# Two searches of a mixture-of-experts kernel placed anew around its first expert

## The reference, cut to what matters

```python
logits = x @ w_gate                      # 3072 tokens, 8 experts
order = np.argsort(-flat)                # all (token, expert) scores, best first
for idx in order:                        # greedy, 384 tokens for each expert
    ...
for e in range(E):
    h = np.maximum(x[mask] @ w1[e], 0.0)     # 320 -> 1024
    out[mask] = h @ w2[e]                    # 1024 -> 320
h = x @ w_in                             # 320 -> 2048
g = np.where(h > 0.0, h, np.exp(np.minimum(h, 0.0)) - 1.0)
return g @ w_out                         # 2048 -> 320
```

## Time and profile before

| | us |
|---|---|
| median of three executions | 812.0 |
| the three | 810.54, 812.0, 812.1 |
| the profiled execution | 811.09 |
| its span in the trace | 809.3 |
| PE, DVE, ACT, POOL busy | 784.3, 520.8, 469.7, 397.2 |
| first expert, layer 1 from block 2 on | 210.07 to 239.96 |
| first expert, layer 2, with blocks 0 and 1 of the second | 239.96 to 295.27 |

### The profile page before, as it was taken

The page is one execution under the profiler, slowest core; times in us unless marked ns, Lnnn a source line. Parts: engine busy times, 40 slices in busy tenths (PEclk is TensorE's granted clock), DMA queues, the critical chain, the costliest instruction groups (busy, mean ns, idle before and its releaser), DMA issues.

```text
span 809.3 us, 17760 instructions
## 1 busy us (share of the span) xinstructions
PE 784.3 (97%) x6063; PEld 727.4 (90%) x6063; DVE 520.8 (64%) x1433; ACT 469.7 (58%) x1003; POOL 397.2 (49%) x472
## 2 busy tenths in 40 slices
PE   8999999999999999999999999999999999999995
PEld 7989898877789989999899999999998999999894
DVE  8667676867669747765865776576658656442441
ACT  7455555412428844882776288448727762993663
POOL 7545555534605750763365166517634651674243
PEclk9999999999999999999999999999999999999998
DMA  8999999333411311222021212112220212221000
GB/s 130 164 152 163 169 169 171 76 95 115 120 47 31 91 41 46 71 60 76 26 65 48 71 48 72 49 41 72 65 70 26 71 48 65 57 63 40 2 1 24
DMA packets 137763, 60.96 MB, mean 75 GB/s; under 512 B 104472, under 2 KB 135960, under 8 KB 137688
## 3 DMA queue, kind: packets, MB, share of 16 engines
q1 hardware_dynamic: 135208, 52.10, 29.7%
q0 software_dynamic: 2464, 7.89, 3.1%
q10 hardware_dynamic: 16, 0.01, 0.0%
HBM read 51.67 MB, written 8.26 MB: 74 GB/s over the span
## 4 chain that ended last, share of the span: by engine, by line
PE 64%; ACT 5%; DVE 4%; POOL 2%; issue 2%; DMA 1%; SPq 1%; ACTq 0%; POOLq 0%
PE bank L1950 7%; PE bank L2045 7%; PE bank L1951 6%; PE bank L1957 6%; PE bank L2047 6%; PE bank L2046 6%; PE bank L1959 3%; PE bank L1958 3%; PE bank L2003 3%; PE bank L2005 3%; PE bank L2004 3%; PE bank L1883 2%; PE bank L1991 1%; PE bank L1988 1%; ACT unit L1803 1%
## 5 line engine op out<-in xcount | busy, mean ns | idle before, releaser
L1359 POOL TENSOR_TENSOR gl_lo<-unit,gl_hi 128x384 fp32r<-128x384 f32 x128 | 130.5, 1020 | 266.3 <-ACT gl_hi L1819 266.1
L2045 PE MATMUL bank<-Wo_hi,gl_hi 128*128 128x320 f32 x384 | 124.8, 325 | 0.6 <-POOL gl_lo L1359 0.6
L2047 PE MATMUL bank<-Wo_hi,gl_lo 128*128 128x320 f32 x384 | 118.6, 309 | 0.0
L2046 PE MATMUL bank<-Wo_lo,gl_hi 128*128 128x320 f32 x384 | 118.3, 308 | 0.0
L1783 ACT ACTIVATE hid_hi<-bank 128x384 fp32r<-128x384 f32 x64 | 31.4, 490 | 129.0 <-PE bank L1959 129.0
L1622 DVE SCALAR_TENSOR_TENSOR unit<-bank,unit 128x384 f32<-128x384 f32 x104 | 57.9, 556 | 73.7 <-ACT bank L1812 73.7
L1800 ACT ACTIVATE unit<-bank 128x384 f32<-128x384 f32 x128 | 62.2, 486 | 49.6 <-PE bank L1959 40.5
L1950 PE MATMUL bank<-x_hi,Wi_hi 128*128 128x384 f32 x224 | 80.2, 358 | 2.4 <-DVE unit L1625 1.6
L1951 PE MATMUL bank<-x_hi,Wi_lo 128*128 128x384 f32 x224 | 75.8, 338 | 0.0
L2045 PEld LDWEIGHTS bank<-Wo_hi,gl_hi 128*128 128x128 f32 x384 | 72.5, 189 | 3.1 <-POOL gl_lo L1359 3.1
L1625 DVE TENSOR_TENSOR unit<-unit,bank 128x384 f32<-128x384 f32 x128 | 70.9, 554 | 4.4
(11 more groups left out here) (301 smaller groups left out, 2098.7 us busy)
## 6 DMA issues: line engine op xcount, KB each, us to landing
stage<-in_moe_w_dram SPq DMA_DIRECT2D x32, 320.0 KB, 2.9
stage<-in_moe_w_dram SPq DMA_DIRECT2D x32, 256.0 KB, 2.6
stage<-in_moe_w_dram SPq DMA_DIRECT2D x96, 64.0 KB, 2.4
k_in<-in_k_dram SPq DMA_DIRECT2D x24, 160.0 KB, 3.8
q_in<-in_q_dram SPq DMA_DIRECT2D x24, 160.0 KB, 4.4
o_in<-in_o_gate_dram SPq DMA_DIRECT2D x24, 160.0 KB, 4.0
v_in<-in_v_dram SPq DMA_DIRECT2D x24, 160.0 KB, 3.6
x_rows<-xt SPq DMA_DIRECT2D x24, 160.0 KB, 3.2
```

Of the source, the lines that this page charges most:

```text
L1359: nc.gpsimd.tensor_tensor(gl_lo[:, b, :], ex[:, b, :], gl_hi[:, b, :].bitcast(F32), ALU.subtract).then_inc(gl_ok, 1)
L2045: nc.tensor.matmul(acc[j][:, 0:DM], gl_hi[:, f % RG, t_], Wo_hi[:, f, :], start=(f == 0), stop=False)
L2046: nc.tensor.matmul(acc[j][:, 0:DM], gl_hi[:, f % RG, t_], Wo_lo[:, f, :], start=False, stop=False)
L2047: return nc.tensor.matmul(acc[j][:, 0:DM], gl_lo[:, f % RG, t_], Wo_hi[:, f, :], start=False, stop=(f == NF2 - 1))
```

## The change

It concerns the first expert alone; it gets a `first_body` of its own on VectorE and on PE, and what the general `body` had for it is deleted.

- Layer 1: each round q = 2 to 6 of the second search lies over block u = q. The threshold product of round u - 1 stands between `up_high(u)` and `up_low(u)`, the count of round u between the first and the second column block of `down(u - 2)` (for which `down` is split into `down_begin` and `down_block`), the fold behind `down`. There are no filler products. `totals` and both `prefix` move to block 7, behind `down(0, 6)` and behind `down(0, 7)`. On VectorE `choose_expert` and `choose_ties` come behind `hidden(0, 7)`, and `choose_leave` and `choose_close` behind `between_layers`.
- Layer 2: `choose_spots` at blocks 0 to 3, `choose_start(2)` at block 4, `list_tokens(1)`, `choose_tokens(1)` and `choose_keys(2)` at block 5, the slices two by two at blocks 6, 7 and 8. The third search goes by half blocks (2f ahead of `down2`, 2f + 1 behind it): round 1 counts at half 21 with its threshold at half 22, and from half 24 on each round has three halves. Round 6 stands at halves 36 and 37, around `down2(0, 15)`. VectorE makes the search's steps ahead of `elu` of the block, and those of round 6's test after `hidden(1, 1)`.

```diff
-    SLICES_BESIDE_SPOTS = {0: (0,), 2: (1,), 4: (2,), 5: (3, 4), 6: (5,)}
+    SLICES_BEHIND_LIST = {6: (0, 1), 7: (2, 3), 8: (4, 5)}
+    LIST_BESIDE, FIRST_LIST_BESIDE = 0, 5
+    def step_beside(half):
+        if half < 24:
+            return {21: (1, 1), 22: (1, 2)}.get(half, (0, 0))
+        return 2 + (half - 24) // 3, (half - 24) % 3
...
@@ VectorE @@
+        def third_search(half):
+            q, part = step_beside(half)
+            if q == 1:
+                if part == 1:
+                    round_test(2, 1)
+                else:
+                    round_move(2, 1)
+                    round_compare(2, 2)
+            elif q in FOLDED:
+                if part == 0:
+                    round_parts(2, q)
+                elif part == 1:
+                    round_test(2, q)
+                else:
+                    round_move(2, q)
+                    round_compare(2, q + 1)
+            elif q == ROUNDS and part == 0:
+                round_test(2, q)
+        def first_body():
+            round_test(1, 1)
+            round_move(1, 1)
+            round_compare(1, 2)
+            hidden(0, 2)
+            for q in range(2, ROUNDS):
+                round_parts(1, q)
+                round_test(1, q)
+                round_move(1, q)
+                round_compare(1, q + 1)
+                hidden(0, q + 1)
+            round_test(1, ROUNDS)
+            round_move(1, ROUNDS)
+            choose_counts(1)
+            hidden(0, NF - 1)
+            choose_expert(1)
+            choose_ties(1)
+            between_layers(0)
+            choose_leave(1)
+            choose_close(1)
+            for f in range(NF2):
+                third_search(2 * f)
+                third_search(2 * f + 1)
+                elu(0, f)
+                if f < SPOTS:
+                    choose_spots(1, f)
+                elif f == SPOTS:
+                    choose_start(2)
+                if f == FIRST_LIST_BESIDE:
+                    choose_tokens(1, 1, 0)
+                    choose_keys(2)
+                for part in SLICES_BEHIND_LIST.get(f, ()):
+                    compare_first(2, part)
+                if TURN <= f < TURN + NJ:
+                    columns(1, f - TURN)
+            for step in range(2):
+                third_search(2 * (NF2 + step))
+                third_search(2 * (NF2 + step) + 1)
+                hidden(1, step)
+            third_search(2 * (NF2 + 2))
+            round_move(2, ROUNDS)
...
@@ TensorE @@
+            elif q in FOLDED:
+                (count_parts, fold_parts, count_thresholds)[part](2, q)
+        def first_body():
+            for u in range(2, NF):
+                up_high(0, u)
+                if u == 2:
+                    count_takers(1, 1)
+                else:
+                    count_thresholds(1, u - 1)
+                up_low(0, u)
+                if u == 2:
+                    count_thresholds(1, 1)
+                down_begin(0, u - 2)
+                if u in FOLDED:
+                    count_parts(1, u)
+                elif u == ROUNDS:
+                    count_takers(1, u)
+                else:
+                    totals(1)
+                down_block(u - 2, 1)
+                if u in FOLDED:
+                    fold_parts(1, u)
+            down(0, NF - 2)
+            prefix(1, 1, eqs)
+            down(0, NF - 1)
+            prefix(1, 2, mem)
+            for f in range(NF2 + LAG):
...
+                third_search(2 * f)
+                if f >= LAG:
+                    down2(0, f - LAG)
+                third_search(2 * f + 1)
+                if f == FIRST_LIST_BESIDE:
+                    list_tokens(1)
+                if TURN <= f < TURN + NJ:
+                    columns(1, f - TURN)
+                if NF2 <= f < NF2 + 2:
+                    up(1, f - NF2)
```

More of the change, by code:

```diff
@@ L1659, in body @@
         def body(k, s, n, after):
+            if first_expert(k):
+                return first_body()
             c = k + 1
             for u in range(2, NF):
[L1663 to L1698, removed]
@@ L1712, in body @@
                 hidden(k, u)
-            if after == 2 and not first_expert(k):
+            if after == 2:
                 choose_start(c + 1)
@@ L1736, in body @@
                     round_test(c + 1, q)
[L1737 removed]
+                if after and f == LIST_BESIDE:
                     choose_tokens(c, 1 - s, n + s)
                 if after == 2:
[L1740 removed]
+                    for part in SLICES_BESIDE.get(f, ()):
                         compare_first(c + 1, part)
[L1742 to L1747, removed]
+                    if f == COUNT_BESIDE:
+                        round_test(c + 1, 1)
                 if TURN <= f < TURN + NJ and after:
                     columns(c, f - TURN)
[L1750 to L1756, removed]
+            if after:
                 hidden(c, 0)
@@ L1978, in up, with down_begin @@
             up_low(k, f)
[L1980 removed]
+        def down_begin(k, f):
             if f == 0:
@@ L2000, in down, with down_block @@
                 ins.then_inc(mid_pe, 1)
[L2001 to L2008, removed]
+            down_block(f, 0)
+        def down_block(f, c):
+            first, last, b, a = f == 0, f == NF - 1, f % HR, c * P
+            nc.tensor.matmul(acc[c][:, 0:CAP], W2[:, f, a:a + P], hid_hi[:, b, :], start=first, stop=False)
+            nc.tensor.matmul(acc[c][:, 0:CAP], W2[:, f, DM + W3 + a:DM + W3 + a + P], hid_hi[:, b, :], start=False, stop=False)
+            ins = nc.tensor.matmul(acc[c][:, 0:CAP], W2[:, f, a:a + P], hid_lo[:, b, :], start=False, stop=last)
+            if last:
+                ins.then_inc(mid_pe, 1)
+            elif c == 1:
                 ins.then_inc(down_pe, 1)
+        def down(k, f):
+            down_begin(k, f)
+            down_block(f, 1)
         def up2(k, f):
@@ L2139, in body @@
                 elif 1 < f < NF2:
-                    if f == LAG and after and not first_expert(k):
+                    if f == LAG and after:
                         list_tokens(c)
```

62 lines of the change are left out of this document (23 added, 39 removed).

## The result

The changed kernel takes 814.3 us in the median of 20 runs (811.6 to 818.7), the kernel before 811.9 us (809.7 to 815.6, 20 runs): a ratio of 1.0030, 95% interval 1.0018 to 1.0043. It is slower by 0.3%; forecast were 809.6 us, 0.3% faster. The profiled execution of after had 814.04 us with a span of 812.3 us, 3.0 us longer than that of before.

What follows compares the result with a forecast made beforehand. PE was taken as the bound, with only avoidable work and waits to win. Layer 1 -3.25, between the layers +0.15 and layer 2 +1.25 sum to -1.85, say -1.9 us: from 811.5 to 809.6 us, range 807.0 to 811.6.

Steps and rivals of the forecast that it cites:

- The waits that appear: Layer 1, blocks 2 to 4: PE waits for VectorE's compares and casts, 0.4, 0.2, 0.3 and 0.1, sum 1.0 us.
- 8.35 - 3.1: Layer 1: 8.35 us of search rounds and slower first products go out, 3.1 us of split small products come back.
- The hold of L1435: Layer 1, block 4: VectorE step held by POOL's split of weight piece 6, delaying compare and count, +1.0 us.
- rival 1: One of two large holds (L1435 in block 4, elu of block 14) is missed: 808.5 us, chance 0.25.
- Between the layers: From layer 1 to layer 2: moved choose steps on VectorE cost PE 0 to 0.6 us, taken as 0.15.
- The weight pieces: Layer 1: the nearest piece is ready 1.0 us before PE wants it, so no wait.
- step (a): Layer 2, blocks 4 and 5: moved key steps held beside POOL for 3 us, 0.4 us of it reaching PE.
- (b): Layer 2, block 16: PE waits 0.5 us at round 4's threshold and 0.8 us for round 5's compare.
- (c): Layer 2, block 14: elu held 1.1 us by POOL's split of piece 5; PE's fold of round 4 waits 1.3.
- The forecast for layer 2: Waits of 1.75 us go, 3.0 us come from key-step holds, block 16 and block 14: net +1.25 us.
- Rival 4: VectorE becomes the bound of blocks 12 to 15, five all-SBUF steps each held 1.1 us: 814.0 us, chance 0.05.
- The sign given for "wrong": Sum wrong if layer 1 gives under 2.5 us, holds are absent, or PE waits over 4 us in blocks 12-16.

Runs made afterwards that it cites:

- layer1_alone: Layer 1 as in the changed kernel, layer 2 and third search as in the kernel before; 811.56 us against 811.06 for before, ratio 1.0004.
- gather_block6: The changed kernel with POOL's three gathers one block earlier (blocks 6 to 8); 809.77 us against 811.53 for the kernel before, ratio 0.9980.
- keys_unheld: The changed kernel with the key steps of blocks 4 and 5 given a PSUM operand; 809.75 us against 811.06 for before, ratio 0.9989.
- after_again: The changed kernel itself, timed again beside the kernel before; 813.65 us against 811.06, ratio 1.0029.
- layer2_alone: Layer 1 as in the kernel before, layer 2 and third search as in the changed kernel; 817.40 us against 811.06 for before, ratio 1.0075.
- fillers_in_wait: The changed kernel with 16 filler products on PE ahead of the count of half block 27; 812.90 us against 811.53 for before, ratio 1.0011.
- split4_later: The changed kernel with POOL's split of weight piece 4 one block later; 812.77 us against 811.53 for the kernel before, ratio 1.0014.
- unheld_split5: keys_unheld with POOL's split of weight piece 5 one block later; 809.08 us against 811.53 for the kernel before, ratio 0.9968.
- gather6_split5: gather_block6 with POOL's split of weight piece 5 one block later; 807.44 us against 811.60 for the kernel before, ratio 0.9955.

## Why the prediction was wrong

**Layer 1: right, but for one hold.** A block with a folded round takes 3.40 us in after (from 222.39 to 225.79), a block without any small product took 2.80 in before (from 233.95 to 236.75): 0.60 for a round, near the 0.57 read from the earlier trace rows. The waits that appear came to about 1.1 us (0.4 and 0.1 in block 2, 0.4 in block 3, 0.2 in block 4) for 1.0 forecast. 8.35 - 3.1 - 1.1 = 4.15, measured 4.14; so close a fit is luck, since the same layer 1 took from 24.50 to 25.45 us in the ten traces that have it (L1; 24.87 in after). The hold of L1435, taken as met at +1.0, was missed:

```profile
220.30 0.18 DVE L1435 SCALAR_TENSOR_TENSOR lo<-hi,lo 128x24 f32<-128x24 f32 x1
...
220.58 1.29 POOL L1067 TENSOR_TENSOR W_split<-stage,W_split 128x512 fp32r<-128x512 f32 x1 [1.20 <-ACT W_split L1051]
```

It is done 0.1 us before POOL starts. In layer1_alone, the same code, the transfers came elsewhere, L1433 took 0.97 and L1435 0.39, and the count waited 0.95. The margin was named (0.2 us), and that is all that can be said of such a hold beforehand; rival 1 (one of the two large holds missed) is what came in layer 1. Between the layers nothing was lost, for 0.15 forecast: from the last product of layer 1 to the first of layer 2 it is 0.47 us in both. The weight pieces cost nothing, as forecast.

**Layer 2, step (a): the size right, the consequence wrong.** The holds of the key steps came to 3.4 us (forecast 3). Four of the eleven steps were held, three with two inputs in SBUF and the cast; the two reductions kept their 0.34 and 0.35 us:

```profile
250.22 1.45 DVE L940 TENSOR_TENSOR score<-L,best 128x192 f32<-128x192 f32 x1
251.70 0.60 DVE L942 TENSOR_TENSOR key<-key_t,best 128x24 int32<-128x24 int32 x1
...
254.55 0.95 DVE L954 CAST hi<-key_hi 128x24 f32<-128x24 int32 x1
...
255.50 1.46 DVE L956 TENSOR_TENSOR pick<-score,top 128x192 bf16<-128x192 f32 x1
```

I compared them with DVE's spare time and let 0.4 us reach PE. The comparison was right as far as it went: DVE made up for the holds by block 11, and they cost PE nothing. But the same holds put off GpSimd's work, and GpSimd has no spare time there: it came to block 12 late by 1.5 us. The failed step is that the sum laid out DVE's queue for blocks 12 to 16 and of POOL's only the split of piece 5, and so did not see that a gather, a split, two `elu_lo` and a further split stand in one train when block 12's `elu` begins.

**The price of a hold: the false assumption.** "So a DVE step without a PSUM operand stands until POOL's running one is done" is the sentence on which all holds were priced, 1.1 us at most. The earlier trace rows bore it out: the step of 276.89 was let in at 277.4 between L1359 and L1067, though a whole train stood there back to back, as POOL's next rows in before show (L1067, beside which the step then ran, takes 1.61 us, a lone one 1.29):

```profile
277.50 1.61 POOL L1067 TENSOR_TENSOR W_split<-stage,W_split 128x512 fp32r<-128x512 f32 x1
279.08 0.45 POOL L1068 TENSOR_TENSOR W_split<-stage,W_split 128x128 fp32r<-128x128 f32 x1
```

In after the same kind of step was passed over at three such borders and lost 3.3 us. The Trainium skill, page "SBUF — State Buffer", section "Summary: rules for kernel authors", says that with two SBUF inputs on VectorE beside a GpSimd step that reads SBUF the second one to issue is blocked until the first finishes. By that the step would have been let in at 271.88, and after would, as an estimate, be a kernel like gather_block6. The trace differs: three more POOL instructions started ahead of the waiting step.

**The clock: a term that was missing.** Nothing in the sum stood for PE's clock. The fall behind the wait of 3.20 us cost 2.7 us more, nearly as much as the wait.

**Steps (b) and (c): right in kind.** Threshold and count in block 16 waited 0.43 and 0.49 to 0.55 in all kernels with the new layer 2 (forecast 0.5 and 0.8), and the hold of block 14's `elu` came, with 1.07 us at the fold, as soon as block 12's was out of the way. In after itself L1435 was held instead (1.23 us), with 1.05 at the count.

**The sum.** The forecast for layer 2 was +1.25 us: gather_block6, which is after without the one hold, has +1.10. Its median was 1.8 us under before, for 1.9 forecast. That fit is in part luck: (a) to (c) were put at 0.4, 1.3 and 1.3 us and came to 0, 0.98 and 1.08, and some 0.5 us came that no term stood for; and the interval of its time reaches from 0.2 to 3.0 us under before. (The second window of the earlier trace rows ends at 294.92, inside the last products; the two blocks end at 295.27. Nothing in the sum hangs on it.) After is that kernel plus 3.2 us of wait and 2.7 us of low clock. Rival 4 had the right place, blocks 12 to 15, and nearly the right time, 814.0 against 814.3; but its mechanism was five steps held once each, and what came was one step held through four POOL steps and one more (L1435) held once, plus the clock. It had 0.05, and its "against" (POOL is idle in part of that stretch) was read off the trace of before, where POOL's phase was another. The sign given for "wrong", over 4 us of waits in blocks 12 to 16, is met: 3.20 + 1.05 + 0.43 + 0.55 = 5.2.

What stays open: why a waiting DVE step was let in at some borders between POOL steps (in after L940 and L956 between the two halves of a split and block 12's `elu` ahead of L1068, in before the `elu` step between L1359 and L1067) and not at three others, one of them again between L1359 and L1067. And some 0.3 to 0.5 us of layer 2 beside waits and clock: gather_block6 is 1.10 us longer than before with 0.60 more of waits.

## What to carry to other kernels

When steps are moved on one engine, lay out the queue of the engine beside which its steps are held as well, over the whole stretch in which the shift lives, and look for trains without a gap: an all-SBUF VectorE step that meets one may pay for the train, not for one step. A delay that the first engine makes good can live on in the second, if that one has no idle time. If a moved step makes a kernel slower, try the other engine's order first: here two moves on GpSimd's queue were worth 6 to 7 us. And where a forecast lets PE wait as long as here (1.97 and 3.20 us), put a stretch of half clock behind the wait, as a term with a chance of its own.

## What the runs showed of the hardware

- A VectorE step of 0.55 us with all operands in SBUF took 3.87, 3.87, 3.86 and 3.89 us in four traces (after, after_again, layer2_alone, fillers_in_wait) beside a train of GpSimd subtractions, and 2.63 us when the train was one split shorter. Where it was let in, the GpSimd step behind it grew (L1068 0.76 us instead of 0.45 in after, L1067 1.61 instead of 1.29 in before).
- The key steps with two inputs in SBUF took 1.45 and 1.46 us beside GpSimd in after; with one operand in PSUM they took 0.34 and 0.35 us in keys_unheld.
- The granted clock fell to 0.50 behind waits of PE of 3.20 us (for 5.8 us) and of 1.97 us (for some 3 us), and stayed at 1.00 behind one of 3.09 us in layer1_alone. Three waits within 4 us, the first of 1.03 to 1.20 and the others of about 0.43 and 0.5 us, stand in seven traces: behind them it fell in keys_unheld (0.52 over 2.8 us) and in fillers_in_wait, and stayed at 1.00 in the other five, gather_block6 with its 1.08, 0.43 and 0.55 us among them. In what the cases differ no row here shows.
- Some executions have the lower clock long before the change: for part of the stretch from 20 to 30 us (mean 0.71 in layer1_alone, 0.73 in split4_later), which puts off the stage by about 5 us, and for part of that from 195 to 200 us (mean 0.71 to 0.79 in fillers_in_wait, gather_block6, unheld_split5 and gather6_split5). A single span is no measure of an edit of 2 us; the stage's own length is.
